# TensorE's program for eight experts: the one-tile body placed ahead of the two-tile body, and the last four hidden transposes waited for in two pairs

## The reference

```python
logits = x @ w_gate                      # 1536 tokens, 8 experts
expert_idx = np.argmax(logits, axis=1)
# each expert takes its tokens in order, at most capacity = 384 of them
h = np.maximum(np.einsum('ecd,edf->ecf', disp, w1), 0.0)   # 512 -> 1024
y = np.einsum('ecf,efd->ecd', h, w2)                       # 1024 -> 512
out[i] = gate_w[i] * y[expert_idx[i], pos[i]]
```

## Time and profile before

| what | value |
|---|---|
| median of 3 runs | 599.58 us (598.77 to 599.89) |
| the profiled execution's own time | 599.18 us |
| its span in the trace | 597.4 us |
| PE busy | 576.2 us (96% of the span) |
| DVE, ACT, POOL busy | 358.2, 269.9, 155.9 us |
| mean granted TensorE clock | 0.992 of full speed |

### The profile page before, as it was taken

How to read it: one execution, slowest core, us unless ns; L and a number is a source line. 1 busy time by engine, 2 the same in 40 slices (tenths; PEclk the granted TensorE clock), 3 DMA queues, 4 the chain that set the end, 5 groups by cost and what they waited for, 6 DMA issues and landing times.

```text
span 597.4 us, 11768 instructions
## 1 busy us (share of the span) xinstructions
PE 576.2 (96%) x3995; PEld 497.3 (83%) x3995; DVE 358.2 (60%) x1061; ACT 269.9 (45%) x672; POOL 155.9 (26%) x253
## 2 busy tenths in 40 slices
PE   8999999999999999999999999998999899899994
PEld 7787888888888888988888899987989789789882
DVE  5878786575556555765566446466639376488310
ACT  6865654343433334433423131134638376498321
POOL 5423542222121222222213100005112235324010
PEclk9999999999999999999999999999999999899997
DMA  7635443001052302010000150026849779789000
GB/s 195 151 97 164 141 116 80 2 19 39 24 172 71 89 19 71 19 37 19 37 8 11 42 171 1 1 83 189 244 177 338 280 198 364 224 285 302 19 25 16
DMA packets 73357, 67.78 MB, mean 113 GB/s; under 512 B 42900, under 2 KB 49060, under 8 KB 73280
## 3 DMA queue, kind: packets, MB, share of 16 engines
q1 hardware_dynamic: 68464, 57.50, 31.0%
q0 software_dynamic: 3760, 9.03, 5.4%
q10 hardware_dynamic: 1056, 0.26, 0.2%
HBM read 58.01 MB, written 12.06 MB: 117 GB/s over the span
## 4 chain that ended last, share of the span: by engine, by line
PE 84%; DVE 6%; issue 4%; ACT 3%; DMA 1%; POOL 0%; SPq 0%; DVEq 0%; POOLq 0%; ACTq 0%
PE bank L1117 22%; PE bank L1119 22%; PE bank L1118 22%; PE bank L1107 9%; PE bank L1161 4%; PE bank L1192 4%; PE bank L1265 1%; ACT wh L807 1%; DVE fw L1747 1%; DVE fw L1752 1%; DMA fw<-y_scratch,mask 1%; DVE wl L1520 1%; DVE fw L1563 1%; DVE rw L1541 1%; DMA o_sb<-in_q_dram 1%
## 5 line engine op out<-in xcount | busy, mean ns | idle before, releaser
L1117 PE MATMUL bank<-rw,wh 128*128 128x256 f32 x512 | 149.2, 291 | 0.0
L1117 PE MATMUL bank<-wh,rw 128*128 128x512 f32 (+1 forms) x368 | 144.9, 394 | 3.4 <-DVE rw L1758 1.6
L1119 PE MATMUL bank<-rw,wl 128*128 128x256 f32 x512 | 144.6, 282 | 0.0
L1118 PE MATMUL bank<-rw,wh 128*128 128x256 f32 x512 | 144.3, 282 | 0.0
L1119 PE MATMUL bank<-wh,rw 128*128 128x512 f32 (+1 forms) x368 | 141.4, 384 | 0.0
L1118 PE MATMUL bank<-wl,rw 128*128 128x512 f32 (+1 forms) x368 | 141.2, 384 | 0.0
L954 ACT CAST rw<-fw 128x256 fp32r<-128x256 f32 x95 | 38.6, 406 | 142.8 <-DVE fw L1752 139.5
L1117 PEld LDWEIGHTS bank<-rw,wh 128*128 128x128 f32 x512 | 97.0, 189 | 2.9 <-DVE rw L1601 0.2
L1118 PEld LDWEIGHTS bank<-rw,wh 128*128 128x128 f32 x512 | 97.0, 189 | 1.7
L1119 PEld LDWEIGHTS bank<-rw,wl 128*128 128x128 f32 x512 | 96.9, 189 | 0.0
L1520 DVE TENSOR_TENSOR wl<-fw,wh 128x512 fp32r<-128x512 f32 x120 | 76.7, 683 | 11.8 <-ACT wh L807 10.7
(11 more groups left out here) (142 smaller groups left out, 692.5 us busy)
## 6 DMA issues: line engine op xcount, KB each, us to landing
fw<-in_moe_w_dram SPq DMA_DIRECT2D x95, 256.0 KB, 5.5
v_raw<-in_moe_w_dram SPq DMA_DIRECT2D x22, 256.0 KB, 5.5
fw<-in_moe_w_in_dram SPq DMA_DIRECT2D x16, 256.0 KB, 3.2
fw<-in_moe_w_out_dram SPq DMA_DIRECT2D x16, 256.0 KB, 2.8
y_scratch<-fw SPq DMA_DIRECT2D x12, 256.0 KB, 2.0
out_dram<-v_or_route SPq DMA_DIRECT2D x12, 256.0 KB, 3.5
v_raw<-in_v_dram SPq DMA_DIRECT2D x11, 256.0 KB, 3.2
o_sb<-in_q_dram SPq DMA_DIRECT2D x11, 256.0 KB, 3.3
```

The lines of the kernel that those rows point to most:

```text
L1117: pe.matmul(dst, ah, bh, start=start, stop=False, skip_group_check=True)
L1118: pe.matmul(dst, ah, bl, start=False, stop=False, skip_group_check=True)
L1119: return pe.matmul(dst, al, bh, start=False, stop=stop, skip_group_check=True)
```

## The change

Three things are written differently in TensorE's program; no other engine's program is touched. `Busy` gets a second test, `within`, the opposite of `over`. The one-tile body, now the function `single_rest`, stands ahead of the two-tile body, and so does `expert_in(first, 0)` ahead of `pair_in(e, 0)`. And `hidden_T(first, 1)` waits for value 3 ahead of its first two transposes, and for value 4 ahead of the last two.

```diff
+            def within(self, e, j):
+                return self.eng.If(self.count[e] < j * P + 1)
...
             def hidden_T(i, c, skipped=0):
                 e, j = ITEMS[i]
-                pe.wait_ge(expert_hidden_by_act, HS * e + (6 + c if j else 1 + 3 * c))
+                pe.wait_ge(expert_hidden_by_act, HS * e + (6 + c if j else 1 + 2 * c))
                 for f in range(NF2 // 2):
+                    if j == 0 and c == 1 and f == NF2 // 4:
+                        pe.wait_ge(expert_hidden_by_act, HS * e + 4)
...
+            def single_rest(e):
+                first = TPE * e
+                hidden_T(first, 0)
+                next_tile(e, 2)
+                next_second_tile(e)
+                single_quarter(first, 0)
+                single_quarter(first, 1)
+                if e + 1 < E:
+                    hidden_T(first, 1, 4)
+                else:
+                    expert_out(first, 2, range(0, 2))
+                    hidden_T(first, 1)
+                    expert_out(first, 2, range(2, NF2))
...
-                with busy.over(e, 1):
+                with busy.within(e, 1):
+                    expert_in(first, 0)
+                with pe.Else():
                     if e == 0:
                         slot_T(1)
                         keep_busy(10, H_BANK[0])
                     pair_in(e, 0)
-                with pe.Else():
-                    expert_in(first, 0)
                 if e:
                     busy.last_of(e - 1, expert_out)
-                with busy.over(e, 1):
+                with busy.within(e, 1):
+                    single_rest(e)
+                with pe.Else():
                     for b in range(1, 4):
                         pair_in(e, b)
...
-                with pe.Else():
-                    hidden_T(first, 0)
-                    next_tile(e, 2)
-                    next_second_tile(e)
-                    single_quarter(first, 0)
-                    single_quarter(first, 1)
-                    if e + 1 < E:
-                        hidden_T(first, 1, 4)
...
```

## The result

The changed kernel takes 602.38 us (median of 7 runs, 601.88 to 603.62), the kernel before 598.61 us (7 runs, 596.26 to 599.89). The ratio is 1.0069, with a 95% interval of 1.0049 to 1.0090: slower by 0.7%.

The account below looks back on a forecast made before the run. PE bounds the kernel, with two issue stalls from late instruction pages. From the profiled 599.18 us, gains of 5.2 and costs of 10.9 gave 604.9, said as 605 us; range 599.8 to 610.5, the forecast's own 601.5 to 608.5.

Parts of the forecast that it names:

- rival 2: Only the two-page jump costs, one-page waits being in time: 600.5, about 601 us against the median; chance 0.09.
- stall of expert 2 gone: Ahead of expert 2's first matmul: expert_in no longer stands behind a page-crossing jump, saving 1.55 us.
- stall of expert 4 and its half clock gone: At expert 4's hidden transposes: stall of 2.02 us and half-clock loss of 1.61 us both disappear.
- two transposes inside ScalarE's wait: Experts 2, 4 and 5: two 0.11 us transposes run during ScalarE's 0.47 us; counted as nothing, bounds 0 to 0.66 gained.
- end of expert 2: Jump from page 30 to 31, entered shortly before, with little cover: adds 1.0 us, bounds 0.4 to 3.5.
- start of expert 3: Jump into page 32 behind pair_in's 24 matmuls, page 31 just entered: adds 1.0 us, bounds 0 to 2.6.
- expert 4 to 5: Page 37 needed after expert 5's expert_in, 2.8 us of matmuls: adds 2.4 us, bounds 0.6 to 5.1.
- end of expert 5: Jump from page 37 to 39, two pages on with nothing queued: adds 4.9 us, bounds 3.2 to 5.6.
- half clock behind it: After the stall at expert 5's end, PE runs at half clock: adds 1.6 us.
- how long until that next page can be used: Delay from entering one instruction page until the next is usable: 4.9 to 8.0 us, from the profile's branches.
- Rival 1: All jumps covered because pages further ahead are already there; only gains count: about 594.2 us; chance 0.11.
- weights are late: Rival in the follow-up runs: late weights or DMA load hold PE, as the profile's releaser says; no chance given.

Follow-up runs that it names:

- 176 dead instructions: Changed kernel with 176 never-executed instructions (88 transposes) in expert 0's unused one-tile body; 611.25 us, ratio 1.0229 to the kernel before.
- expert 5 pair-first: Changed kernel with expert 5 alone in the old order, two-tile body ahead of the one-tile body; 599.80 us, ratio 1.0020 to the kernel before.
- expert 4 alone: Kernel before's order of bodies except expert 4, which has the one-tile body first; changed kernel's split waits and first-product order kept; 601.06 us, ratio 1.0049.
- the run with 10 transposes: Changed kernel with 10 useless transposes queued ahead of the long jump at expert 5's end; 602.63 us, ratio 1.0051 to the kernel before.
- the tail apart: Changed kernel with a one-tile expert's last four hidden transposes moved behind both bodies, under their own test; 599.36 us, ratio 1.0021 to the kernel before.
- the last run: Two-tile body cut in three with one-tile parts between, plus 100 never-executed instructions in expert 4's last_of; 598.57 us, ratio 1.0018 to the kernel before.
- the 80 dead instructions: Changed kernel with last hidden transposes behind both bodies, plus 80 never-executed instructions in expert 4's last_of; 598.01 us, ratio 0.9978 to the kernel before.
- the bodies in three parts: Changed kernel with the two-tile body cut in three, one-tile parts between, last transposes behind all; 598.09 us, ratio 0.9970 to the kernel before.

## Why the prediction was right or wrong

Right: that it is slower, and where most of the time is lost. 602.4 us lies within the range (599.8 to 610.5) and within the forecast's own (601.5 to 608.5), 2.6 us under the 605 named. But it lies nearer to rival 2 (only the jump of two pages costs, 601), and the terms say why.

Term by term, with what the changed kernel's trace has:

| term | predicted | measured |
|---|---|---|
| stall of expert 2 gone | -1.55 | -1.7 |
| stall of expert 4 and its half clock gone | -3.6 | -3.5 |
| two transposes inside ScalarE's wait | 0 | -0.2 in expert 2 (that of expert 4 is in the row above) |
| end of expert 2 | +1.0 | +0.4 |
| start of expert 3 | +1.0 | 0 (branch 1.8 us, covered) |
| expert 4 to 5 | +2.4 | +0.7 (0.44 of it idle time) |
| end of expert 5 | +4.9 | +5.5 |
| half clock behind it | +1.6 | +2.2 |

The second row's measured value is the step from -1.41 to -4.91 in the table of starts; it includes two transposes saved and the 0.25 us at the jump. That of expert 4 to 5 is the step from -4.91 to -4.19. In all the sum had +5.7 us and the trace has +3.5.

The step that was mis-sized is "how long until that next page can be used". I took 4.9 to 8 us, from the branches of 522.2 and 526.4 and of 497.4 and 501.3. In the changed kernel the page after that of 517.9 was usable at 521.5, 3.6 us; and page 31 cost nothing at the end of expert 2, though I had it asked for 4.1 us before: its packet started at 477.29, 3.9 us before the jump, and landed at 478.25. So three terms of 1.0, 1.0 and 2.4 us came to 0.4, 0 and 0.7, 3.3 us less. That is what rival 2 says of the one-page waits, here; where a page is entered shortly before its end they cost 2.5 to 3.7 us, as with 176 dead instructions, with expert 5 pair-first and with expert 4 alone. The two terms for expert 5 were 1.2 us too small together. The half clock lasted 6.8 us and not 3.4, the first 1.8 us of it while PE still stood idle: I had carried the length over from a stall of 2.0 us to one of 5.5. That the total is only 2.2 us off is in part luck, since these errors go against each other. The branch at the end of expert 2, for which I named 0.5 to 4 us as a sign, took 0.39.

The sequencer's lead was 15 to 17 matmuls at the long branches that no wait and no other branch stood shortly ahead of, and the run with 10 transposes and the one with the tail apart show that it is what makes a jump cheap or dear. Why a one-tile body first is worse, then: not for the length of its jump, which is the same, but because it stands behind `hidden_T`'s wait, where the queue is empty. Rival 1 (all covered) fell with the branch of 532.0, and "weights are late" with the dead instructions.

Of my own expectations three were plainly too hopeful (expert 5 pair-first, expert 4 alone, the last run) and that with the 80 dead instructions somewhat, all for one reason: I counted the stall that was removed and took the pages behind it to arrive as they had, or nearly.

The packets of instructions say how such a time is made up, which the branches alone don't. In all 14 traces the experts' parts have 69 branches of over 0.6 us, and each ends 1.27 to 1.55 us after a packet of 16 KB has landed. Some of them:

| trace | branch | its packet | packet's start after the branch's | branch's end after the landing |
|---|---|---|---|---|
| changed kernel | 532.00 to 537.45 | 535.12 to 536.13 | 3.1 | 1.3 |
| changed kernel | 518.50 to 521.47 | 518.88 to 520.14 | 0.4 | 1.3 |
| before | 509.74 to 515.68 | 513.35 to 514.28 | 3.6 | 1.4 |
| before | 526.36 to 527.07 | 524.62 to 525.65 | -1.7 | 1.4 |
| before | 575.15 to 578.65 | 576.15 to 577.28 | 1.0 | 1.4 |
| tail apart | 528.75 to 535.19 | 532.89 to 533.85 | 4.1 | 1.3 |

The packet itself takes 0.9 to 1.4 us. What differs is the time before it starts. Five long jumps stand in the last expert, where the DMA engines are idle: their packets start 0.97 to 1.01 us after the branch. In experts 2 to 6, where the engines are busy from the branch's start to the packet's for a share of 0.35 to 1.12, it is 1.0 to 4.1 us. So my 4.9 and 5.7 us were true waits, and the error was to carry them over to another place as one fixed delay.

Open: what sets that time. It goes with the load on the DMA engines, but not evenly (1.3 us at a share of 1.12 with the tail apart and 80 dead instructions, 3.6 us at 0.83 before), and no run here changed the load alone. That the next page is asked for on entry fits (the packet of 518.88 comes 1.0 us after the jump of 517.50 ended), but the trace shows the packet and not the asking.

## What to carry to other kernels

In a program with branches on data, put a long jump where its engine has the most work queued, and never right behind a wait that empties the queue; the body that is jumped over is best cut so that no jump is longer than a page, which was worth 1% here against the changed kernel and 0.3% against before, and the 0.3% went again with 100 dead instructions. Look at the branches' own durations before believing a releaser: an idle time that ends with a branch of several us isn't a late operand. And measure an edit's neighbours: with pages of 256 instructions, any added or removed instruction ahead moves every boundary behind it, and two versions that differ in dead code alone were 1.6% apart.

## What the runs showed of the hardware that I had not expected

- Straight code can stall for its page: 3.65 us between two neighbouring matmuls without a wait (530.76 to 534.70) in the run with expert 5 pair-first, 3.5 us in that with expert 4 alone, 2.53 us with 176 dead instructions. It happened where a jump had entered the page before only 2 to 6 us earlier.
- The jump into another page wasn't free even with everything there: 0.29 to 0.43 us, against 0.17 to 0.23 us within a page and 0.07 us for a branch not taken.
- A branch that waits for its page ends 1.3 to 1.5 us after the packet of 16 KB has landed (69 branches), and between its start and that packet's up to 4.1 us pass.
- Half clock, 1.2 instead of 2.4 GHz, was granted for 3.4 us with idle times of 2.0, 2.5, 3.2 to 3.5 and 3.9 us, for 6.8 us with 3.7, 4.4 and 5.5 to 5.7 us, and not at all with 0.95 to 1.9 us. But it wasn't granted with 2.6 us either, in the profile of the bodies in three parts, and 3.9 us brought less of it than 3.7: the length of the idle time alone doesn't decide it.
